# Three-stage attention and mixtures: split first logits, scanned ranks, tap band laid out by the host, gate products between chunks, a seam that loads before its tables

## What is computed

```python
def reference(**kwargs):
    attn_out = _attn_ref(**attn_kwargs)       # per head: out[s] = sum_k softmax(weight)[k] * x[s - 6 + k]
    x = attn_out.reshape(B * S, D)            # 14336 tokens of 192 numbers
    x = _moe_ref(x=x, **moe_kwargs)           # logits = x @ w_gate (8 experts), the best expert alone
    return _moe2_ref(x=x, **moe2_kwargs)      # noisy logits, the two best experts, weighted sum
...
# an expert: h = np.maximum(xe @ w1[e], 0.0); ye = h @ w2[e]     (192 -> 1024 -> 192)
```

## Time and profile before

| what | value |
|---|---|
| median of 3 runs | 2104.25 us (2103.11 to 2105.91) |
| the profiled execution's own time | 2097.81 us |
| its span | 2096.1 us |
| busy: PE, DVE, ACT, POOL | 1930.1, 1263.6, 902.5, 907.4 us |
| mean granted clock of PE over the span | 0.963 of full |
| stage A, start to the first matmul of the first mixture | 255.92 us |
| second seam, first matmul of the second mixture | 952.86 us |

### The profile page before, as it was taken

How to read it: one execution, slowest core, us unless ns; L and a number is a source line. 1 busy time by engine, 2 the same in 40 slices (tenths; PEclk the granted TensorE clock), 3 DMA queues, 4 the chain that set the end, 5 groups by cost and what they waited for, 6 DMA issues and landing times.

```text
span 2096.1 us, 50969 instructions
## 1 busy us (share of the span) xinstructions
PE 1930.1 (92%) x14215; PEld 1857.0 (89%) x14216; DVE 1263.6 (60%) x4287; ACT 902.5 (43%) x2390; POOL 907.4 (43%) x1175
## 2 busy tenths in 40 slices
PE   6677489999999999988999999999999999999998
PEld 4555388988999989988999999999999999999998
DVE  5323457777677776775555565555555655555555
ACT  2222235455455454553444444444444444444444
POOL 4555523333333333334444444444444444444444
PEclk9877599999999999998999999999999999999999
DMA  6343233233232332323223222232232222322321
GB/s 217 127 131 123 62 93 107 84 104 106 80 113 81 101 106 80 108 70 104 61 64 94 62 76 81 63 101 62 66 98 60 78 81 62 99 62 67 94 63 49
DMA packets 113593, 185.37 MB, mean 88 GB/s; under 512 B 21548, under 2 KB 89636, under 8 KB 111392
## 3 DMA queue, kind: packets, MB, share of 16 engines
q1 hardware_dynamic: 73120, 104.74, 16.6%
q0 software_dynamic: 40320, 79.90, 12.0%
q10 hardware_dynamic: 128, 0.46, 0.1%
HBM read 111.73 MB, written 77.40 MB: 90 GB/s over the span
## 4 chain that ended last, share of the span: by engine, by line
PE 61%; another core or an unknown queue 10%; issue 10%; DVE 8%; DMA 4%; ACT 4%; SPq 2%; DVEq 1%; ACTq 1%; POOL 0%; POOLq 0%
PE bank L1087 19%; PE bank L1088 9%; PE bank L1072 6%; PE bank L1068 6%; PE bank L1070 6%; PE bank L1071 5%; PE bank L1069 5%; DMA rows<-rows_of_mixture 4%; DVE h_l L808 2%; ACT h_h L534 2%; PE bank L935 1%; PE bank L1057 1%; ACT x_in L553 1%; DVE x_h L769 1%
## 5 line engine op out<-in xcount | busy, mean ns | idle before, releaser
L1087 PE MATMUL bank<-w2hl,h_h 128*128 128x384 f32 (+1 forms) x2832 | 866.1, 370 | 45.4 <-DVE h_l L808 45.1
L1088 PE MATMUL bank<-w2hl,h_l 128*128 128x192 f32 (+1 forms) x2832 | 721.4, 255 | 0.0
L808 DVE SCALAR_TENSOR_TENSOR h_l<-bank,h_h 128x512 fp32r<-128x512 f32 x708 | 478.5, 688 | 228.1 <-ACT h_h L534 184.0
L534 ACT ACTIVATE h_h<-bank 128x512 fp32r<-128x512 f32 x708 | 421.6, 596 | 416.6 <-PE bank L1072 252.9
L1087 PEld LDWEIGHTS bank<-w2hl,h_h 128*128 128x128 f32 x2832 | 534.1, 189 | 57.7 <-DVE h_l L808 56.2
L1088 PEld LDWEIGHTS bank<-w2hl,h_l 128*128 128x128 f32 x2832 | 543.3, 192 | 0.0
L1187 POOL DMA_INDIRECT rows_of_mixture<-x_in,pos x248 | 242.1, 976 | 446.8 <-DVE pos L856 379.7
L1068 PE MATMUL bank<-x_h,w1mh 128*128 128x256 f32 x1416 | 402.4, 284 | 11.8 <-DVE x_h L769 11.8
L1071 PE MATMUL bank<-x_h,w1lh 128*128 128x256 f32 x1416 | 400.9, 283 | 0.0
L1070 PE MATMUL bank<-x_h,w1ml 128*128 128x256 f32 x1416 | 400.9, 283 | 0.0
L1072 PE MATMUL bank<-x_h,w1ll 128*128 128x256 f32 x1416 | 398.9, 282 | 0.0
(11 more groups left out here) (182 smaller groups left out, 1903.2 us busy)
## 6 DMA issues: line engine op xcount, KB each, us to landing
rows<-rows_of_mixture SPq DMA_DIRECT2D x179, 208.0 KB
raw<-in_w_of_both SPq DMA_DIRECT2D x17, 1024.0 KB
raw<-in_w_of_both SPq DMA_DIRECT2D x17, 768.0 KB
x_in<-in_x SPq DMA_DIRECT2D x16, 768.0 KB
out<-zeros SPq DMA_DIRECT2D x61, 192.0 KB
rows_of_mixture<-pad_rows SPq DMA_DIRECT2D x20, 208.0 KB, 9.5
rows_of_mixture<-x_in,pos POOLq DMA_INDIRECT x248
so_far<-out,at_n POOLq DMA_INDIRECT x232
```

The source lines that it names most:

```text
L534: nc.scalar.activation(h_h[:, 2 * p:2 * p + 2, :].rearrange("p c t -> p (c t)"), bank[1 + p][:], ACT.Relu).then_inc(hh_ready[m], 1)
L808: V.scalar_tensor_tensor(h_l[:, 2 * p:2 * p + 2, :].rearrange("p c t -> p (c t)"), bank[1 + p][:], 0.0, h_h[:, 2 * p:2 * p + 2, :].rearran ...
L1087: T.matmul(dst, h_h[:, c, tok], both, start=(c == 0), stop=False)
L1088: last = T.matmul(bank[5 + a][:, 0:width], h_l[:, c, tok], w2hl[:, c, 0:width], start=False, stop=(c == F // P - 1))
```

## The change

The tap band. The host lays each head's seven raw taps on the diagonals of a 128 by 112 matrix, all other places hold the first tap, and the array comes in by a DMA on ACT's queue. The device subtracts each head's maximum, takes the exponential and multiplies by a 0/1 band (`keep`) over the sum, in two halves. Before, DVE and POOL built the band with 7 shifted identities.

The first logits. ACT copies all three groups of transposed tokens as rounded `fp32r` numbers, DVE subtracts to get the remainders (`lanes_split`), and six matmuls replace three. The gate holds its high and low half as separate columns, so that there are 64 rows of logits instead of 128, and DVE adds the halves.

The ranks. One scan on DVE (`seen`) counts the experts over the tiles of a chunk, so two matmuls replace nine.

The copies. DVE's `conv_out` does one of its two copies, ACT's new `conv_last` the other.

The gate products. `fold` 0 to 3 move from the start to steps 1, 2, 4 and 5, and 4 to 7 to 8, 9, 10 and 12. Their loads move behind the first chunks.

The seams. The first weights are split in steps 11 to 15. SP loads the first slot before the tables are known, a memset on POOL marks each landed chunk (`landed`), and a slot's readiness is one register load and one wait, taken before the wait for the rows' buffer. DVE does the first slot's split and capture before it loads the total into a register. `tables` has three operations less.

```diff
-FOLD_BEFORE_RANKS = {2: 4, 5: 5, 8: 6, 11: 7}
-LOADS_AFTER = {9: 5, 12: 6, 15: 7}
+FOLD_BEFORE_RANKS = {1: 0, 2: 1, 4: 2, 5: 3, 8: 4, 9: 5, 10: 6, 12: 7}
+TURNED_AFTER = {8: 2, 9: 3, 11: 4, 12: 5, 14: 6}
+FOLD_ACROSS_AT, FOLD_TURN_AT, FOLD_OUT_AT = {5: 0, 12: 1}, {6: 0, 13: 1}, {6: 0, 13: 1}
+W1_HIGH_AT, W1_LOW_AT, W2_HIGH_AT = 11, 12, {15: (0, 1)}
...
+            load_chunk(0)
+            sp_.dma_start(g1_in[:].rearrange("p k e -> p (k e)"), gate1).then_inc(gates_in, 16)
             for i, g in enumerate((gate2, gate_noise)):
                 sp_.dma_start(g2[:].rearrange("p k (h g) -> p (k h) g", h=2)[:, :, i * E:(i + 1) * E],
                               g.rearrange("p (k e) -> p k e", e=E)).then_inc(fold_gates_in, 16)
-            for e in range(FOLD_FIRST):
-                load_turned(e)
-            load_chunk(0)
-            sp_.dma_start(g1s[:].rearrange("p k e -> p (k e)"), gate1).then_inc(gates_in, 16)
             for c in range(1, XIN):
...
                 load_chunk(c)
-                if c in LOADS_AFTER:
-                    load_turned(LOADS_AFTER[c])
+                if c in TURNED_AFTER:
+                    load_turned(TURNED_AFTER[c])
+            sp_.wait_ge(folded, 6)
+            load_w1(0)
+            load_turned(E - 1)
             sp_.wait_ge(folded, E)
-            load_w1(0)
             load_w2(0)
 
...
+                sp_.wait_ge(pads_known[m], 1)
+                pad(0)
                 sp_.wait_ge(tables_ready[m], 1)
+                sp_.wait_ge(padded[m], 16)
                 with sp_.Fori(0, E) as e:
                     start, more = slots_of(sp_, m, e)
                     pad(e + 1)
                     with sp_.Fori(0, more + 1) as j:
-                        until((xt2_done[m], start + j + 1),
-                              (captured[m], start + j + 1))
                         with sp_.If(j < more):
...
                 if c + 1 < CHUNKS:
                     lanes_out(c + 1)
+                shifted_exp(c)
+                if c + 1 < CHUNKS:
                     other_columns(c + 1)
-                shifted_exp(c)
                 if c + 2 < CHUNKS:
-                    low_pairs(c + 2)
-            fold_across(1)
-            fold_out_of(1)
-            for p in range(PAIRS):
-                split_w1_h(0, p)
-            for p in range(PAIRS):
-                split_w2_h(0, p)
-            split_gates_h(slice(0, 1))
+                    conv_last(c + 2)
+                if W1_HIGH_AT <= c < W1_HIGH_AT + PAIRS:
+                    split_w1_h(0, c - W1_HIGH_AT)
+                if c in FOLD_ACROSS_AT:
+                    fold_across(FOLD_ACROSS_AT[c])
+                if c in FOLD_OUT_AT:
+                    fold_out_of(FOLD_OUT_AT[c])
+                for p in W2_HIGH_AT.get(c, ()):
+                    split_w2_h(0, p)
 
...
+            for heads in halves:
+                V.tensor_tensor(band[:, heads], band[:, heads], bc(tap_max[:, heads].unsqueeze(2), some), ALU.subtract).then_inc(band_shifted, 1)
...
+            for half, heads in enumerate(halves):
+                link(V.tensor_tensor(band_w[:, heads], bc(keep[:].unsqueeze(1), some), bc(tap_div[:, heads].unsqueeze(2), some), ALU.mult))
+                dve.wait_ge(band_exped, half + 1)
+                V.tensor_tensor(band[:, heads], band[:, heads], band_w[:, heads], ALU.mult).then_inc(band_ready, 1)
...
-            for heads in (range(HEADS // 2), range(HEADS // 2, DVE_HEADS)):
-                for k in range(TAPS):
-                    for h in heads:
-                        if k == 0:
-                            last = V.tensor_scalar(band[:, h, :], shift[:, k, :], tap_w[:, h, k:k + 1], None, ALU.mult)
-                        else:
-                            last = V.scalar_tensor_tensor(band[:, h, :], shift[:, k, :], tap_w[:, h, k:k + 1], band[:, h, :],
-                                                          ALU.mult, ALU.add)
-                    if k < TAPS - 1:
-                        link(last)
-                last.then_inc(band_ready, 1)
...
+            def lanes_split(c):
                 dve.wait_ge(logits_done, c)
-                V.tensor_copy(xt_odd[:], bank[5][:, 0:HALF]).then_inc(odd_ready, 1)
+                dve.wait_ge(even_ready, c + 1)
+                V.tensor_tensor(xl_even[:], bank[4][:, 0:HALF], xh_even[:], ALU.subtract).then_inc(even_split, 1)
+                dve.wait_ge(low_ready, c + 1)
+                V.tensor_tensor(xl_low[:], bank[6][:, 0:HALF], xh_low[:], ALU.subtract).then_inc(low_split, 1)
+                dve.wait_ge(odd_ready, c + 1)
+                V.tensor_tensor(xl_odd[:], bank[5][:, 0:HALF], xh_odd[:], ALU.subtract).then_inc(odd_split, 1)
...
+                halves = bank[2][0:TILE, 0:RANKS].rearrange("p (t w) -> p t w", w=4 * E)[:, :, 0:2 * E].rearrange("p t (h e) -> p t e h", h=2)
+                link(V.reduce_sum(c_lg[:], halves, AX.X))
+                link(V.reduce_max(c_max[:], c_lg[:], AX.X))
...
+                link(V.tensor_tensor(c_mask, c_val[:], bc(c_best[:].unsqueeze(2), full), ALU.is_equal))
+                flat = [t[:].rearrange("p e t -> p (e t)") for t in (seen, carry, seen_in)]
+                V.tensor_tensor_scan(flat[0], flat[1], flat[2], 0.0, ALU.mult, ALU.add).then_inc(mask_ready, 1)
...
-                link(V.tensor_tensor(c_rank[:], bank[2][0:TILE, RANKS:RANKS + CHUNK * E].rearrange("p (t e) -> p t e", e=E),
-                                     bc(ecap[0:TILE, :].unsqueeze(1), full), ALU.add))
+                ranks = bank[2][0:TILE, RANKS:RANKS + CHUNK * E].rearrange("p (t e) -> p t e", e=E)
+                link(V.scalar_tensor_tensor(c_at[:], ranks, float(E * CAP), c_mask, ALU.add, ALU.mult))
...
+            def place_first(c, link):
                 link(V.reduce_sum(c_posf[:], c_at[:], AX.X))
-                link(V.reduce_sum(c_new[:], c_mask[:].rearrange("p t e -> p e t"), AX.X))
-                link(V.tensor_tensor(count1[:], count1[:], c_new[:], ALU.add))
-                V.tensor_copy(c_pos[:, c % XROW, :], c_posf[:]).then_inc(pos_ready, 1)
+                link(V.tensor_copy(seen_in[:, :, 0:1], seen[:, :, CHUNK:CHUNK + 1]))
+                V.scalar_tensor_tensor(c_pos[:, c % XROW, :], c_best[:], -float(CAP), c_posf[:], ALU.mult, ALU.add).then_inc(pos_ready, 1)
...
+                if W1_LOW_AT <= c < W1_LOW_AT + PAIRS:
+                    split_w1_l(0, c - W1_LOW_AT)
+            last_chunk = link
...
+                T.matmul(logits, g1s[:, 0, :], xl_even[:], start=False, stop=False)
+                pe.wait_ge(low_split, c + 1)
+                T.matmul(logits, g1s[:, 2, :], xl_low[:], start=False, stop=False)
+                pe.wait_ge(odd_split, c + 1)
+                T.matmul(logits, g1s[:, 1, :], xl_odd[:], start=False, stop=True).then_inc(logits_done, 1)
...
-                T.matmul(ranks, before[0:TILE, 0:TILE], c_mask[:].rearrange("p t e -> p (t e)"), start=True, stop=False)
-                for j in range(CHUNK - 1):
-                    n = CHUNK - 1 - j
-                    T.matmul(bank[2][0:TILE, RANKS + (j + 1) * E:RANKS + CHUNK * E].rearrange("p (t e) -> p t e", e=E),
-                             ones_b[0:TILE, 0:TILE], bc(c_mask[:, j:j + 1, :], [TILE, n, E]), start=False, stop=False)
+                T.matmul(ranks.rearrange("p (t e) -> p t e", e=E), before[0:TILE, 0:TILE], c_mask, start=True, stop=False)
                 T.matmul(ranks.rearrange("p (t e) -> p t e", e=E), ones_b[0:TILE, 0:TILE],
-                         bc(count1[:].unsqueeze(1), [TILE, CHUNK, E]), start=False, stop=True).then_inc(rank_done, 1)
+                         seen[:, :, 0:CHUNK].rearrange("p e t -> p t e"), start=False, stop=True).then_inc(rank_done, 1)
...
-            fold_turn(1)
-            pe.wait_ge(pos_ready, CHUNKS)
             for m in range(2):
...
+            def mark_landed(c):
+
+                pool.wait_ge(scattered1[c % XROW], 16 * CHUNK * (c // XROW + 1))
+                G.memset(landed_mark[:, c:c + 1], 0.0).then_inc(landed, 1)
```

More of the change, by code:

```diff
@@ L11 @@
 GROUP = D // HEADS
-DVE_HEADS = 6
 N = BATCH * SEQ
@@ L332, in all_scattered @@
                 def all_scattered():
[L333 to L334 removed]
+                    sp_.wait_ge(landed, CHUNKS)
                 def slot_scattered(j):
[L338 to L340 removed]
+                    v = sp_.value_load(due[0:1, bass.ds(j, 1)], min_val=EARLY_AT[0], max_val=CHUNKS)
+                    until((landed, v))
                 def all_sent():
@@ L374, in _ @@
                             else:
-                                with sp_.If(e * WORD + j >= EARLY_2 - 1):
+                                with sp_.If(e * WORD + j >= EARLY_ROWS[1] - 1):
                                     all_sent()
+                            until((xt2_done[m], start + j + 1),
+                                  (captured[m], start + j + 1))
                             load_rows(e * CAP + j * SLOT + SLOT)
@@ L382, in _ @@
                                 all_sent()
```

(23 more changed lines are left out.)

300 lines of the change are left out of this document (156 added, 144 removed).

## The result

The changed kernel took 2129.54 us (median of 4 runs, 2124.91 to 2141.84) against 2103.72 for the kernel before on the same chip: 1.0131 times as long, with a 95% interval of 1.0105 to 1.0158. That is 26 us slower, where 2075 us, 29 us faster, had been forecast, and it lies outside the range.

What follows compares the result with a forecast made beforehand. The loop was taken as a chain over all engines, the mixtures as PE-filled. Terms -10 - 9 - 4.6 - 5 - 1 = -29.6 gave 2068 us profiled, 2075 us median (own range 2060 to 2090; range 2032 to 2099).

Steps and rivals of the forecast that it cites:

- The start, -10: Up to chunk 0 placed: the tap band is ready sooner, first convolution at about 13 us, 10 us earlier.
- The loop, -9: Loop over chunks: PE's net -12 us against 3 us charged for DVE and ACT, so 9 us shorter.
- PE's -12: PE in the loop: cheaper logits and rank matmuls, less added gate products and `fold_turn`, net 12 us saved.
- the 3 us charged: Added DVE and ACT work in the loop, mostly covered by DVE's waits: 3 us charged, 11 if uncovered.
- The seam, -4.6: First seam, last ranks to first expert matmul: 7.9 us against 12.5 without the unexplained wait, 4.6 us saved.
- the waits of the earlier trace: DVE's unexplained waits in the loop, more than 72 us; rival: they go, giving 2030 us, chance 0.18.
- The early slots, -5: From 256 to 345 us: 5 of PE's 8.3 us of waits for late rows are saved.
- the second seam, -1: Second seam: three operations less and the first slot's split no longer behind the register load, 1 us saved.
- The clock did not fall: Rival: less PE work lowers PE's clock in the loop; below 0.60 the kernel is slower, 2119 us at 0.55; chance 0.08.

Runs made afterwards that it cites:

- the last experiment: Kernel with 33 memsets, without the three matmul passes over the tokens' low parts in the first router's logits: 1931.62 us for 1932.73, loop 110.23 us instead of 115.32.
- 33 memsets: Changed kernel with 33 one-element memsets at the start of DVE's program, moving its later instructions 33 places down: 1932.73 us against 1956.41 for the kernel before, ratio 0.987.

## Why the prediction was wrong

**What failed is the step that isn't in the sum.** The change was costed part by part, and every part counted only the instructions it runs. "The mixtures fill PE with matmuls that the diff leaves alone, so what can be won lies in the first 345 us and at the second seam": that sentence held for gains and not for losses. The diff took 33 instructions from DVE's program ahead of the expert loop and so moved the loop over a block's edge. The sum had nothing for this; it cost 49 us of waits on the first chip, and 49 of waits and 56 of time on the others. The counts of instructions were to be had ahead of the run (not which places are bad, which took the experiments), and the 17 instruction packets of the kernel before could have been read as a loop that stays in the engine. No rival named it either.

**The start, -10.** Right: -8.8, and -10.7 on the other chip. The first product of the band was ready about when forecast (PE's first convolution starts at 12.23 us), the second half's convolution started at 16.15 us and not at 13, 1.05 us of it a wait for ACT's copy of the first half; chunk 0 then needed 15.5 us, not 17.4. Two errors that nearly cancel.

**The loop, -9.** -8.2 on the first chip, -1.3 on the other. The mechanism was right and the prices of the logits on PE too: the three passes of before fill 2.34 us at full clock on the other chip, six passes now 1.3. What was mis-sized is PE's -12. It was priced at the first chip's clock of 0.76; where the clock is near full, PE's busy time in the loop fell by 4.8 us only (112.67 to 107.90). And it was taken whole, where the last experiment shows that about half of PE's relief is won: by these two numbers some -2.4, an estimate. DVE's busy time in the loop rose by 12.7 us and ACT's by 17.4; from -2.4 to the measured -1.3 some 1 us is left for them, so that the 3 us charged were not too few. The agreement on the first chip is in part luck: its loop holds stops that differ between the two executions.

**The seam, -4.6.** Right in mechanism where nothing else stops DVE: -6.4, and 4.66 us from placing to matmul. On the first chip it was +7.6, through the late starts shown above. The same instructions in the same places took 4.66 us on the other chip, so neither the change nor the place in the program is enough to explain them. That they belong with the waits of the earlier trace rows is likely and not shown.

**The early slots, -5, and the second seam, -1.** The waits of the earlier trace rows are gone: PE waits for no row between 256 and 345 us in the changed kernel. The first mixture and the second seam gave -4.4 us on the other chip. On the first it is less sure: with the 49 us of DVE's waits taken off the +41.2 it is -7.8, with the 54 us by which the seven slots grew it is some -12. On the other chips the two slots at the second seam take 24.7 us with 33 memsets and 23.6 before, so the last -1 did not come.

**The rivals.** The waits of the earlier trace rows neither went nor grew by the change (67.4 us for 72.3 on the first chip); they went with the chip. The clock did not fall: 0.79 in the loop, 0.76 before. Without DVE's stalls the kernel has 0.987 of the time of before, which would be 2077 us for 2104.25; the forecast was 2075. No such kernel ran on the first chip, and the nearness is in part luck: the gain on the other chip was 23.7 us (1956.41 to 1932.73), and the terms of its ledger are not those of the forecast. The version with 33 memsets beats both kernels on the chips that ran it and is the one to keep; a form that puts the branch for single slots behind both loops may do as well and wasn't tried.

**What stays open.** What stops PE, DVE and ACT together in stage A and at the seam on the first chip isn't known. The longest stretch in which none of the three works is 7.8 us before (235.5 to 243.4 us) and 9.7 changed (123.2 to 132.9), while POOL goes on with its DMAs, so it isn't the whole core that stands. It wasn't seen on three other chips and so couldn't be tried. That the engine keeps a fixed number of blocks and fetches one ahead of need is argued from the counts. Shown is that length and place decide, and the rule of blocks of 128 fits every row of the table.

## What to carry to other kernels

Code that runs once can have a price where it stands ahead of a long loop: here its length decided over how many blocks of instructions DVE's loop lay. Before a change is judged, compare the number of instruction packets and the "issue" waits at the loop's head in both profiles; where they differ, a few idle instructions in a wait, or rare branches moved out of the loop, settle in one run whether the change or its place is slow. And a profile of one chip gives the size of a term only for that chip's clock and stops.

## What the hardware showed

In the changed kernel a jump back to the head of the badly placed loop costs DVE 7.4 to 9.0 us in place of some 1.05, with four packets of 8 KB in 6 to 9 us and a fifth about one slot earlier; in the experiments with a bad place such a jump costs 6.5 to 11.4. The Trainium skill, Runtime: NRT & Kernel Launch, Instruction fetch mechanics, says that most engines hold 32 KiB (512 instructions), refilled in blocks of 16 KiB, and that a taken branch out of the current window forces a fetch before execution goes on. The traces agree with the last part. They differ on the block: the packets of that queue have 8 KB, not 16 (PE's, on the other queue, have 16), and the good and bad places fit blocks of 128 instructions, not 256. And a loop of 294 instructions, under the 512 of the skill's section, is fetched again at some places and not at others: fitting in size is not enough.

Instructions that are never executed can cost: 100 of them in a branch of the loop made the kernel before 3.6% slower, and 82 taken out made the changed one 3% faster (by their ratios to the kernel before, one run each).

The same kernel, the one before, took 2104 us on one chip and 1956 to 1958 on three others. Most of the difference lies in the loop of stage A (204.2 us at a clock of 0.76 against 116.7 at 0.99), the rest nearly all in the slots of the first mixture, 10.8 us against 10.0 to 10.1.
